# Probabilities by values: four 128x128 products per step, or eight 64x64 ones into two halves of the partitions

## The reference

```
scores = q @ k.T / 8;  keep 0 <= i - j < 64;  attn = softmax(scores);  o = attn @ v      # per batch and head
x  = o laid out as 2304 x 512
xn = x / rms(x) * rms_g;  x2 = (silu(xn @ w_gate) * (xn @ w_val)) @ w_out                  # width 1536
h  = x2 @ w_in;           out = (h * sigmoid(1.702 h)) @ w_out2                            # width 2048
```

## Time and profile before

| | us |
|---|---|
| median of 3 runs | 980.57 (978.93 to 983.12) |
| the profiled execution | 981.89 |
| its span, first to last instruction | 980.1 |
| TensorE products busy | 946.6 (97%) |
| VectorE busy | 406.0 (41%) |
| ScalarE busy | 357.9 (37%) |
| GpSimd busy | 109.1 (11%) |

### The profile page before, as it was taken

The page is one execution under the profiler, slowest core; times in us unless marked ns, Lnnn a source line. Parts: engine busy times, 40 slices in busy tenths (PEclk is TensorE's granted clock), DMA queues, the critical chain, the costliest instruction groups (busy, mean ns, idle before and its releaser), DMA issues.

```text
span 980.1 us, 12296 instructions
## 1 busy us (share of the span) xinstructions
PE 946.6 (97%) x4750; PEld 798.3 (81%) x4750; DVE 406.0 (41%) x735; ACT 357.9 (37%) x747; POOL 109.1 (11%) x159
## 2 busy tenths in 40 slices
PE   4589999999999999999999999999999999999998
PEld 3489888888888888888888888888888888888897
DVE  1479754444444444443434454224223322422332
ACT  2266655444545345553411122223222222321232
POOL 4446400110010100101012220000000000000000
PEclk7599999999999999999999999999999999999999
DMA  4466311210222102210122323002000100100010
GB/s 134 133 193 202 122 57 57 68 58 11 78 68 70 44 11 89 70 44 11 43 93 82 114 78 108 1 1 87 1 1 35 51 1 1 65 1 1 0 44 22
DMA packets 33420, 57.56 MB, mean 59 GB/s; under 512 B 3409, under 2 KB 9041, under 8 KB 33361
## 3 DMA queue, kind: packets, MB, share of 16 engines
q1 hardware_dynamic: 33360, 56.77, 18.1%
HBM read 47.32 MB, written 9.44 MB: 58 GB/s over the span
## 4 chain that ended last, share of the span: by engine, by line
PE 91%; DVE 3%; issue 3%; POOL 2%; ACT 1%; POOLq 0%; DVEq 0%
PE ps L437 21%; PE ps L439 21%; PE ps L438 21%; PE ps L536 7%; PE ps L535 7%; PE ps L537 7%; PE ps L427 3%; PE ps L404 3%; PE ps L417 1%; DVE w_all L725 1%; PE ps L400 1%; ACT prob L556 1%; PE ps L434 1%; POOL sq L353 0%; DVE nmax L679 0%
## 5 line engine op out<-in xcount | busy, mean ns | idle before, releaser
L437 PE MATMUL ps<-x_hi,w_all 128*128 128x512 f32 (+1 forms) x800 | 301.7, 377 | 4.2 <-DVE x_lo L715 3.7
L439 PE MATMUL ps<-x_lo,w_all 128*128 128x512 f32 (+1 forms) x800 | 295.8, 370 | 0.0
L438 PE MATMUL ps<-x_hi,w_all 128*128 128x512 f32 (+1 forms) x800 | 295.3, 369 | 0.0
L437 PEld LDWEIGHTS ps<-x_hi,w_all 128*128 128x128 f32 x800 | 152.0, 190 | 29.1 <-issue 4.4
L439 PEld LDWEIGHTS ps<-x_lo,w_all 128*128 128x128 f32 x800 | 151.6, 189 | 25.9
L438 PEld LDWEIGHTS ps<-x_hi,w_all 128*128 128x128 f32 x800 | 152.0, 190 | 24.2
L812 DVE TENSOR_TENSOR hid<-ps,sig 128x512 f32<-128x512 f32 (+1 forms) x80 | 51.1, 638 | 208.0 <-ACT sig L642 207.8
L642 ACT ACTIVATE sig<-ps 128x512 f32<-128x512 f32 (+1 forms) x80 | 44.5, 556 | 215.8 <-PE ps L439 215.8
L535 PE MATMUL ps<-w_all,h_hi 128*128 128x512 f32 x288 | 112.2, 390 | 0.0
L536 PE MATMUL ps<-w_all,h_hi 128*128 128x512 f32 x288 | 112.2, 390 | 0.0
L537 PE MATMUL ps<-w_all,h_lo 128*128 128x512 f32 x288 | 112.0, 389 | 0.0
(11 more groups left out here) (71 smaller groups left out, 999.5 us busy)
## 6 DMA issues: line engine op xcount, KB each, us to landing
qbd<-in_q_bd SPq DMA_DIRECT2D x36, 256.0 KB, 2.7
wstage<-in_w_a SPq DMA_DIRECT2D x36, 256.0 KB, 3.2
vwin<-in_v_win SPq DMA_DIRECT2D x36, 256.0 KB, 2.7
wstage<-in_w_b SPq DMA_DIRECT2D x32, 256.0 KB, 3.0
kwin<-in_k_t SPq DMA_DIRECT2D x36, 160.0 KB, 2.8
out_dram<-late SPq DMA_DIRECT2D x18, 256.0 KB, 2.7
xT<-x_scratch SPq DMA_DIRECT2D x4, 1024.0 KB, 5.8
x_scratch<-wstage SPq DMA_DIRECT2D x3, 1024.0 KB, 4.2
```

Source lines behind the costliest of these rows:

```text
L437: pe.matmul(out_, w[:, 0, cols], xh, start=first, stop=False)
L438: pe.matmul(out_, w[:, 1, cols], xh, start=False, stop=False)
L439: return pe.matmul(out_, w[:, 0, cols], xl, start=False, stop=last)
```

## The change

Each block's product becomes two, one per head: 64 columns of `vwin` as weights, the head's 64 columns of `probT` as the moving operand. Head 0's result goes to partitions 0 to 63, head 1's to 64 to 127, both to the same 64 columns of the bank, so the four blocks fill 256 columns of all 128 partitions and nothing that isn't wanted is computed. One ScalarE copy of 128x256 takes the output, where it stood before. VectorE's copy is left out, and with it one of two semaphores; those who waited for both wait for the one.

```diff
-        o_evacuated = [sem(f"o_evacuated{h}") for h in range(2)]
+        o_evacuated = sem("o_evacuated")
...
-        def evacuate_o(eng, copy, h, s):
-            t, c, at_, dst, src = o_half(h, s)
+        def evacuate_o(eng, copy, s):
+            t, c, at_ = home_of(s)
             eng.wait_ge(pv_done, s + 1)
             wait(eng, x_hi_ready, DC * t)
             wait(eng, x_lo_ready, DC * t)
-            copy(dst, src).then_inc(o_evacuated[h], 1)
+            copy(xT[:, c, at_:at_ + GT], ps[:, o_bank(s), 0:GT]).then_inc(o_evacuated, 1)
...
             def squares(s):
-                for h in range(2):
-                    pool.wait_ge(o_evacuated[h], s + 1)
+                pool.wait_ge(o_evacuated, s + 1)
...
             def transpose_probs(s):
                 else:
-                    for h in range(2):
-                        pe.wait_ge(o_evacuated[h], s)
+                    pe.wait_ge(o_evacuated, s)
...
             def probs_by_v(s):
                 if s < EARLY:
+                    wait(pe, o_evacuated, s - 1)
+                for i in range(GB):
                     for h in range(2):
-                        wait(pe, o_evacuated[h], s - 1)
-                for i in range(GB):
-                    ins = pe.matmul(ps[:, o_bank(s), i * P:(i + 1) * P], vwin[:, s % 2, i * P:(i + 1) * P],
-                                    probT[:, i * P:(i + 1) * P], start=True, stop=True)
+                        cols = slice(i * P + h * BLK, i * P + (h + 1) * BLK)
+                        ins = pe.matmul(ps[h * BLK:(h + 1) * BLK, o_bank(s), i * BLK:(i + 1) * BLK],
+                                        vwin[:, s % 2, cols], probT[:, cols], start=True, stop=True)
                 ins.then_inc(pv_done, 1)
...
-                    evacuate_o(act, nc.scalar.copy, 1, s - 1)
+                    evacuate_o(act, nc.scalar.copy, s - 1)
...
                 reciprocal_of_sum(s)
-                if s >= 1:
-                    evacuate_o(dve, nc.vector.tensor_copy, 0, s - 1)
                 evacuate_probT(s)
-            evacuate_o(dve, nc.vector.tensor_copy, 0, EARLY - 1)
             weights_lo_A(0)
...
                     hid_lo_A(t, c)
-                    if first <= s - 1 < last:
-                        evacuate_o(dve, nc.vector.tensor_copy, 0, s - 1)
                     if t == 0 and c + 2 < CA:
                         weights_lo_A(c + 2)
```

More of the change, by code:

```diff
@@ L177, in x2stage, with home_of @@
             return home[:, 0:DC * TMAX].rearrange("p (c t) -> p c t", c=DC)
-        def o_half(h, s):
-            rows = slice(h * BLK, (h + 1) * BLK)
+        def home_of(s):
             group, c = divmod(s, PAIRS)
             t = 0 if group == 0 else (group + 1) // 2
-            at_ = group * GT - TILES_A[t][0]
-            src = ps[rows, o_bank(s), :].rearrange("p (n k) -> p n k", n=GB)[:, :, h * BLK:(h + 1) * BLK]
-            return t, c, at_, xT[rows, c, at_:at_ + GT].rearrange("p (n r) -> p n r", n=GB), src
-        def evacuate_o(eng, copy, h, s):
-            t, c, at_, dst, src = o_half(h, s)
+            return t, c, group * GT - TILES_A[t][0]
+        def evacuate_o(eng, copy, s):
+            t, c, at_ = home_of(s)
             eng.wait_ge(pv_done, s + 1)
@@ L339, in squares @@
             def squares(s):
-                t, c, at_, _, _ = o_half(0, s)
+                t, c, at_ = home_of(s)
                 group = s // PAIRS
                 done = SQ * group
-                for h in range(2):
-                    pool.wait_ge(o_evacuated[h], s + 1)
+                pool.wait_ge(o_evacuated, s + 1)
                 x = xT[:, c, at_:at_ + GT]
```

## The result

| | before | changed |
|---|---|---|
| median of 9 runs each | 981.83 us | 976.72 us (975.74 to 977.24) |
| ratio to before | 1 | 0.9949, 95% interval 0.9940 to 0.9959 |
| the profiled execution, its span | 981.89, 980.1 | 976.94, 975.1 |

What follows compares the result with a forecast made beforehand. TensorE, busy 97% of the span, was taken as the bound, with waits counting before 127 us. Full-clock blocks 5.8, low-clock blocks 1.8 and VectorE's room 3.1 made 10.7 us off 981.9: 971 us, range 963 to 992.

Steps and rivals of the forecast that it cites:

- early, VectorE's room: Before the first tile: VectorE's splits finish before GpSimd's squares start, so the squares take 0.61 instead of 2.20; gain 1.6 us.
- early, four blocks: Four low-clock blocks of probabilities by values go from 1.84 to 1.40 us each; gain 1.8 us.
- first tile, VectorE's room: First tile: VectorE, without its copy and its wait for the products, shortens TensorE's stalls; gain 1.5 us.
- first tile, eight blocks: First tile's eight full-clock blocks of probabilities by values go from 0.88 to 0.70 us each; gain 1.4 us.
- late, 24 blocks: Late steps' 24 full-clock blocks of probabilities by values go from 0.88 to 0.70 us each; gain 4.3 us.
- the 2.2: First tile: TensorE's stalls for transposed probabilities and squares, together 2.2 us, of which 1.5 was taken as gain.
- stalls under 1 us in all between 66 and 118 us: Sign expected in the profile after: TensorE's first-tile stalls sum to under 1 us, showing the first tile's gain.
- the row of a block after a stall: Block from 64.22 us, 1.09 against 1.00 without a stall: 0.09 us taken per change of mode, 0.18 a block.
- the rival with dear changes: Halves overlap but each change of mode costs 0.265 us, a full-clock block 1.05; 984 us, chance 0.12.
- the copy's price on ScalarE: ScalarE's output copy of 128 partitions takes 0.360 us, no more than 0.368 for 64, so ScalarE pays nothing.
- the squares of 0.61 us in the early stage: GpSimd's squares at about 36 to 38 us take 0.61 instead of 2.20 us, all on the chain.
- the rival without overlap: Sixteen pairs run one after another, 1.10 us a block; slower than before beyond 0.98; likeliest 987 us, chance 0.35.

Runs made afterwards that it cites:

- e3: Changed kernel's products with the copies of before: VectorE copies 64 partitions of the output and ScalarE the other 64; 975.95 us, ratio 0.9942.
- e5: Changed kernel plus one wait: in the first tile GpSimd takes a step's squares only after VectorE's weight splits of the same chunk; 972.53 us, ratio 0.9911.
- e1: Changed kernel with each block's eight products reordered, four of head 0 and then four of head 1; 983.88 us, ratio 1.0028.
- e6: Kernel before plus one wait: in the first tile GpSimd's squares come after VectorE's weight splits of the same chunk; 980.32 us, ratio 0.9990.
- e9: Same kernel as e3 (new products, both engines copy), run again beside the changed kernel on the same chip; 975.99 us, ratio 0.9947.

## Why the prediction was right and wrong

By its own steps, the gain in us:

| step | predicted | measured | from |
|---|---|---|---|
| early, VectorE's room | 1.6 | 1.4 | first product, e3 44.01 to changed 42.60 |
| early, four blocks | 1.8 | 2.2 | first product, before 46.22 to e3 44.01 |
| first tile, VectorE's room | 1.5 | -2.1 | first tile, e3 70.2 to changed 72.3 |
| first tile, eight blocks | 1.4 | 1.1 | first tile, before 71.3 to e3 70.2 |
| late, 24 blocks | 4.3 | 2.3 | 350.78 to 348.46, of it 24 x 0.083 = 2.0 |
| sum | 10.7 | 4.9 | spans: 5.0 |

**The step that failed** is VectorE's room in the first tile: "I take 1.5 of the 2.2", with ends 0 and 2.2 and so no loss. The sign is wrong. The prediction had both facts in hand: squares and splits slow each other, and VectorE's order changes when they meet. It used this in the early stage, where the splits move clear of the squares, and did not ask in the first tile where they move to. There the copy had been what made VectorE come first in half of the steps. e3 against the changed kernel shows it twice (2.1 and 1.4 us), e5 takes the contention away and gets 4.2 us. The prediction's own sign, stalls under 1 us in all between 66 and 118 us, came out as 5.1 (0.33, 0.78, 1.27, 0.88, 0.80 and 1.02 before the products). Of the 5.7 us between the forecast and the spans, 3.6 lie in this step and 2.0 in the late blocks.

**The term that was mis-sized** is the late block, 0.70 us predicted and 0.81 measured. The overlap was right and even a little better than foretold (eight slots of 0.0585 and not nine, 0.47 against 0.52, since a head's first product doesn't wait for the other head's second record). The changes of mode were put at 0.18 us a block, by the row of a block after a stall, and are 0.346, halfway from there to the 0.53 of the rival with dear changes. The nearest row was no good measure, as after a stall only the load is bare, and here something at the other end is too (the load behind starts 0.156 us after the last pair). Over 24 blocks that is 4.0 us, less the 1.2 won by the better overlap, and less 0.4 because the block of before costs 0.90 us in a late step and not the 0.88 read in the first tile; together some 2.4, which leaves 24 x 0.083 = 2.0 of the 4.3 forecast. From the block's first record to the second product behind it are 0.95 us and not 0.82.

**What was right**: what bounds each stage; the copy's price on ScalarE; the squares of 0.61 us in the early stage; that halves overlap, on which the forecast's sign hung. The turning point of the rival without overlap, 0.98 us a block, was not right for its reason: it counted on the 3.1 us of VectorE's room, of which nothing was left in sum. e1 has just the 1.10 us a block of that rival and takes 983.9, slower than before but not the 987 it gave. In the rival with dear changes the low-clock part is off by its own terms: 1.84 less 9 x 0.115 + 2 x 0.265 is 0.27 us a block, 1.1 gained and not 0.4, so 983 and not 984.

**A smaller thing at the early blocks**: each goes from 1.84 to 1.05 us (15.15 to 16.20), 0.79 and not the 0.44 predicted, so four should give 3.2 us, and the 2.2 measured, near the 1.8 forecast, are luck in part. The missing microsecond doesn't need the shorter blocks as its cause: it comes and goes between executions. The scores of step 3 take 1.41 us in the profile of before and 1.91 in the changed kernel's for the same eight records, but 1.91 also in e6, which up to there is the program of before:

```profile
26.42 1.41 PE L404 MATMUL ps<-kwin,qbd 128*128 128x128 f32 x8
```

```profile
24.86 1.91 PE L400 MATMUL ps<-kwin,qbd 128*128 128x128 f32 x8 [0.33 <-issue]
```

```profile
26.60 1.91 PE L406 MATMUL ps<-kwin,qbd 128*128 128x128 f32 x8 [0.22 <-issue]
```

The granted clock from 12 to 46 us is 0.57 in the profile of before, 0.54 in the changed kernel's and 0.52 in e6's. In the first of them it had risen from the 1.2 GHz level to 2.4 during these scores, in the other two it hadn't. From e6's first product (47.20) to e3's and e9's (44.01 and 43.89) are 3.2 and 3.3 us, what the four blocks should give.

## What to carry to other kernels

Two products into the two halves of the partitions do run at once, if they alternate; but each trip from the whole array to halves and back costs 0.34 us at full clock here, so put as many half-array products as can be between two changes of mode (here four pairs of products a trip won 0.08 us; by these prices, an estimate, one pair, saving 0.11 us of work against 0.34, would lose). When an instruction is taken off an engine, ask what each instruction behind it now meets on the other engines: here, in the first tile, a copy that cost VectorE 0.34 us kept GpSimd's squares behind its splits in half of the steps, and removing it cost more than it gave. Look in the engine's order for a gap that a movable instruction fills; one split moved and one wait added brought 976.7 us down to 969.8, more than the change itself.

## What the runs showed of the hardware that was not expected

- Half-array float32 products start two at a time, 7 ns apart, every 0.0585 us, although each head's two records stand together in the program: so the second head's first record overtakes the first head's second one. This is inferred, since records don't name the head: e1 rules out that the two of a pair are one product's. In e1 head 1 starts 0.29 us after head 0, with three of head 0's eight records still to come.
- Whole array to halves and back: 0.346 us at full clock with 16 or 32 half-array records in between, 0.34 with 4.
- A VectorE subtraction with two SBUF inputs takes 0.68 us alone and 1.10 to 1.22 behind a running GpSimd instruction; GpSimd's squares take 0.61 alone and 2.20 when they start behind the first of three such subtractions: they are let in only behind the last.
- The same early program ran with first products 1.0 us apart (46.22 and 47.20, before and e6), at granted clocks of 0.57 and 0.52 over 34 us: a microsecond of early gain can't be read from one pair of profiles.
